# Attention and two expert networks on one core: first scores and last evictions moved across the branch, masks in two parts, three products moved between the last turns and values

## The chip, the cores and the metric

The kernel runs on one core of one Trainium2 chip. The time is device microseconds (us) of one execution; the smaller the better. TensorE is called PE here, its weight loads PEld, VectorE DVE, ScalarE ACT, GpSimd POOL and SyncE SP, as in the profile.

## What is computed

The input is q, k, v (2 batches, 8 heads, 768 positions, 64 per head) and the weights of two networks. The first stage is attention in which a row sees the first `n_sink` = 4 positions and the last `window` = 128; the second is a gated network of width 2048, the third a mixture of 4 experts of width 1024, all in float32.

```
keep = is_sink | ((rel >= 0) & (rel < window))
scores = np.where(keep, scale * q @ k.T, -1e9); a = exp(scores - max); a /= a.sum()
x = (a @ v) as 1536 tokens x 512
h = x @ w_in;  g = h * tanh(log1p(exp(h)));  x = g @ w_out
out = sum over 4 experts of p[:, e] * (relu(x @ w1[e]) @ w2[e])
```

## The kernel before

Every engine has a program of its own, written out by hand; semaphores tie them. All engines first run a short setup, then read a flag (`value_load`) that DVE computes from `n_sink` and `window`, and branch: the windowed attention (taken here) or a general one. Each path ends with its own copy of `networks`.

**Attention.** Two heads at a time (`ct` = 0 to 3) are worked in 24 units: unit u is one head's scores of 128 query rows in one batch. Four units make a group g (0 to 5 in a `ct`), so there are 24 groups. A unit passes PE (`score_of`, into one of four banks, `UP_BANK + u % 4`), DVE (`mask_scores`, adds the mask and finds the row minimum), ACT (`exponent`), and by groups DVE (`invert`), POOL (`normalise`), PE (`turn`, transposes), ACT (`copy_first`) and DVE (`copy_second`), PE (`values`), ACT and DVE (`take`: the result as a high part `x_hi` and a rest `x_lo`). PE's program for a period is scores of group g, `values` of group g - 3, `turn` of group g - 2. The first two query blocks of a batch need masks of 128 and 256 columns, the others 272 columns, in an even and an odd kind.

**First network.** PE makes 32 steps `up` (12 products of 128x512, 4 for each of three high/low combinations) and `down` (12 more) per 512 tokens and pass. Step s passes a chain of DVE and ACT between them: `start_gate` (DVE), `exponential` (ACT), `square` (DVE), `reciprocal` (ACT, two instructions), `finish_first` and `finish_second` (DVE, four instructions, the last counted by `g_done`), `gate_hi` (ACT), `gate_lo` (DVE, counted by `mish_lo`). `down` of step s waits for `mish_lo` s + 1. PE runs three `up` ahead (`LAG`); the first three are `start_up(0..2)`, made in the attention's code between the last groups, and `networks` begins with

```
                pe.wait_ge(x_lo_done, X_DONE)
                chunk(0, 0, False)
```

that is, a wait for the last `take` of the attention, then the fourth `up`. ACT's program after its last exponents is in this order: `copy_first` of group 4 of the last `ct`, three instructions that split weight tiles 3 and 4, `exponential(0)`, `take` of group 4, `copy_first` of group 5, `reciprocal(0)`, `take` of group 5; then `networks`, which splits tile 5 and then runs `gate_hi(0)`. DVE's is: `copy_second` 4, `start_gate(0)`, `square(0)`, `take` 4, `copy_second` 5, `finish_first(0)`, `finish_second(0)`, `start_gate(1)`, `take` 5, and in `networks` `gate_lo(0)`, `square(1)`, `start_gate(2)`.

**Experts.** PE alternates products (`L813`) and `tile_down` (`L887`); DVE's `evict` (L1673) adds a tile to the output's sum, six tiles in TILE_ORDER per step. Tile k may be written when the eviction of tile k - 4 is done. SP sends each of the last tiles out as soon as it is evicted, and waits for all of them.

## Time and profile before

| | us |
|---|---|
| median of 3 runs | 859.29 (858.17 to 859.41) |
| the profiled execution's own time | 859.52 |
| its span | 857.7 |
| PE busy | 844.3 (98%) |
| DVE busy | 606.3 (71%) |
| ACT busy | 401.9 (47%) |
| POOL busy | 169.3 (20%) |
| granted TensorE clock, mean | 0.999 |

The span begins with the first instruction and ends with the last; the time of a run is 1.82 us more than the span. The attention ends at about 97 us, the first network at about 360 us. Busy shares are averages over stages with different limits, so the stage in question has to be read by itself. In a timeline row the first number is the start, the second the duration, and in brackets stands how long the engine was idle before it and what the profile names as having ended that.

### The profile page before, as it was taken

The numbers are of one execution on the slowest core, as the hardware profiler recorded it, in microseconds if no ns is written. First come the engines' busy times: TensorE is split into PE (matmuls) and PEld (weight loads), VectorE is DVE, ScalarE is ACT, GpSimd is POOL, SyncE is SP. The second block draws the span as 40 slices with busy tenths as digits, with TensorE's granted clock in tenths as the row PEclk, the third lists the DMA queues.
The fourth block names the chain that finished last, engine by engine and source line by source line (L and its number), as shares of the span: only waits on it lengthen the run. The fifth ranks groups of instructions, "written<-read, shape, count | busy, mean of one in ns | idle before, by whom it ended". The sixth has DMA issues, their size and how long they took to land.

```text
span 857.7 us, 13864 instructions
## 1 busy us (share of the span) xinstructions
PE 844.3 (98%) x4512; PEld 730.1 (85%) x4512; DVE 606.3 (71%) x1173; ACT 401.9 (47%) x739; POOL 169.3 (20%) x255
## 2 busy tenths in 40 slices
PE   6999999999999999999999999999999999999997
PEld 4777888888888888899998999889989998899886
DVE  6888699888888989876566565565565655656655
ACT  5999764447754548754224324314314423432310
POOL 4777300001100112222022012112202202202100
PEclk9999999999999999999999999999999999999999
DMA  7355640003850005734055045135225315403303
GB/s 255 120 152 169 170 101 1 0 1 74 196 124 0 0 0 107 165 72 91 27 118 115 17 100 116 34 82 116 52 64 116 69 47 116 95 24 65 68 9 142
DMA packets 25191, 72.72 MB, mean 85 GB/s; under 512 B 4288, under 2 KB 5952, under 8 KB 25152
## 3 DMA queue, kind: packets, MB, share of 16 engines
q0 software_dynamic: 10720, 33.82, 21.8%
q1 hardware_dynamic: 14288, 38.04, 12.9%
q10 hardware_dynamic: 144, 0.39, 0.1%
q8 instruction: 17, 0.28, 0.1%
q14 instruction: 22, 0.18, 0.1%
HBM read 35.28 MB, written 3.15 MB: 45 GB/s over the span
## 4 chain that ended last, share of the span: by engine, by line
PE 97%; DVE 1%; ACT 1%; DMA 1%; issue 0%; DVEq 0%; ACTq 0%
PE banks L887 31%; PE banks L813 27%; PE banks L784 15%; PE banks L606 15%; PE banks L687 3%; PE banks L660 2%; PE banks L621 2%; PE banks L693 1%; DMA prm<-params 1%; ACT pool L982 0%; ACT prob_third L982 0%; DVE pool L1402 0%; PE banks L663 0%; DVE mask L1313 0%; DVE pool L1673 0%
## 5 line engine op out<-in xcount | busy, mean ns | idle before, releaser
L1673 DVE SCALAR_TENSOR_TENSOR pool<-banks,p_norm,pool 128x512 f32<-128x512 f32 x180 | 133.5, 748 | 66.7 <-PE banks L887 65.0
L887 PE MATMUL banks<-w_hi,g_lo 128*128 128x512 f32 x384 | 150.7, 392 | 0.0
L887 PE MATMUL banks<-w_lo,g_hi 128*128 128x512 f32 x384 | 150.5, 392 | 0.0
L887 PE MATMUL banks<-w_hi,g_hi 128*128 128x512 f32 x384 | 149.3, 389 | 0.0
L1203 ACT ACTIVATE g_hi<-pool 128x384 fp32r<-128x384 f32 x96 | 50.5, 526 | 190.8 <-DVE pool L1653 139.2
L813 PE MATMUL banks<-x_hi,w_lo 128*128 128x384 f32 x256 | 86.0, 336 | 0.0
L813 PE MATMUL banks<-x_hi,w_hi 128*128 128x384 f32 x256 | 85.9, 335 | 0.0
L813 PE MATMUL banks<-x_lo,w_hi 128*128 128x384 f32 x256 | 85.7, 335 | 0.0
L887 PEld LDWEIGHTS banks<-w_hi,g_lo 128*128 128x128 f32 x384 | 72.0, 188 | 15.1
L887 PEld LDWEIGHTS banks<-w_lo,g_hi 128*128 128x128 f32 x384 | 72.1, 188 | 13.9
L887 PEld LDWEIGHTS banks<-w_hi,g_hi 128*128 128x128 f32 x384 | 72.1, 188 | 13.6
L1197 ACT ACTIVATE g_hi<-banks 128x384 fp32r<-128x384 f32 x32 | 15.7, 491 | 131.4 <-PE banks L813 131.4
L519 POOL DMA_DIRECT2D w_lo<-w_sum x15 | 13.1, 875 | 323.3 <-ACT w_lo L1113 323.3
L784 PE MATMUL banks<-g_hi,w_hi 128*128 128x512 f32 x192 | 75.4, 393 | 0.2 <-DVE g_lo L1532 0.2
L606 PE MATMUL banks<-x_hi,w_hi 128*128 128x512 f32 (+1 forms) x192 | 75.0, 391 | 0.0
L784 PE MATMUL banks<-g_hi,w_lo 128*128 128x512 f32 x192 | 74.8, 390 | 0.0
L784 PE MATMUL banks<-g_lo,w_hi 128*128 128x512 f32 x192 | 74.8, 390 | 0.0
L606 PE MATMUL banks<-x_lo,w_hi 128*128 128x512 f32 (+1 forms) x192 | 74.8, 389 | 0.0
L606 PE MATMUL banks<-x_hi,w_lo 128*128 128x512 f32 (+1 forms) x192 | 74.7, 389 | 0.0
L1660 DVE SCALAR_TENSOR_TENSOR g_lo<-pool,g_hi 128x384 fp32r<-128x384 f32 x96 | 53.2, 555 | 21.6 <-ACT g_hi L1203 17.8
L959 ACT ACTIVATE pool<-pool,two 128x512 f32<-128x512 f32 x48 | 34.8, 724 | 69.9 <-DVE pool L1370 69.9
L1631 DVE TENSOR_TENSOR pool<-banks,pool 128x384 f32<-128x384 f32 x32 | 17.8, 557 | 53.6 <-ACT pool L1132 44.5
(142 smaller groups left out, 1770.0 us busy)
## 6 DMA issues: line engine op xcount, KB each, us to landing
w_raw<-weights SPq DMA_DIRECT2D x48, 512.0 KB, 4.3
w_lo<-w_raw POOLq DMA_DIRECT2D x48, 512.0 KB, 5.4
w_lo<-w_sum POOLq DMA_DIRECT2D x15, 384.0 KB, 4.0
pool<-kT SPq DMA_DIRECT2D x8, 400.0 KB, 5.1
pool<-v SPq DMA_DIRECT2D x8, 384.0 KB, 3.2
out<-pool SPq DMA_DIRECT2D x12, 256.0 KB, 2.2
pool<-qT SPq DMA_DIRECT2D x7, 384.0 KB, 4.2
w_lo<-pool POOLq DMA_DIRECT2D x2, 384.0 KB, 4.9
```

Source lines behind the costliest of these rows:

```text
L606: mm = pe.matmul(banks[:, 4 + f % H_RING, :], w[:, f, k * P:(k + 1) * P], x[:, k, ds(c * CHUNK, CHUNK)], start=(k == 0 and n == 0), stop=( ...
L621: mm = pe.matmul(bank[:, col:col + n], q_pair[rows, b, j * P:(j + 1) * P], k_pair[rows, b, key:key + n], start=True, stop=True)
L660: mm = pe.transpose(banks[:, TURN_BANK + n, P * (2 * h + k):P * (2 * h + k) + P], window_prob(u + h, WIDE)[:, col:col + P], ident[:, :])
L687: mm = pe.matmul(banks[D * h:D * h + D, out_bank, column], v_pair[:, b, kt, D * h:D * h + D], prob_T[:, slot, P * (2 * h + k):P * (2 * h + ...
L784: mm = pe.matmul(banks[:, i, :], w[:, f, lo:hi], g_slot(h, g), start=(f == 0 and n == 0), stop=(f == STEPS - 1 and n == 2), skip_group_che ...
L813: mm = pe.matmul(banks[:, bank, 0:HALF], w_cols(w, p2 * SLOT + at + k * P, P), x_part(lo, s, name)[:, k * HALF:(k + 1) * HALF], start=(fir ...
L887: mm = pe.matmul(banks[:, bank, :], g[:, s, f * SUP + at:f * SUP + at + P], w_cols(w, p2 * SLOT + DOWN_AT[f], DM), start=(f == 0 and n == ...
L959: act.activation(r_buf[:, s % 2, :], n_buf[:, s % 2, :], ACT.Ln, bias=two[:, 0:1]).then_inc(l_done, 1)
L1203: act.activation(relu_of(s, f, l), source, ACT.Relu).then_inc(relu_hi, 1)
L1631: dve.tensor_tensor(c12, bank(5 + s), p1_sum, ALU.add).then_inc(sum_done, 1)
L1660: dve.scalar_tensor_tensor(out=g_lo[:, s, at], in0=source, scalar=0.0, in1=g_hi[:, s, at].bitcast(f32), op0=ALU.max, op1=ALU.subtract).the ...
L1673: dve.scalar_tensor_tensor(out=to, in0=d_bank, scalar=share, in1=to, op0=ALU.mult, op1=ALU.add)\
```

## The change

Start. The first key and query loads of batch 0 are split: the first 256 columns of each on a semaphore `qk_first`, the rest on `qk_in[0]`. PE makes the scores of units 0 to 3 before it reads the flag, instead of after the branch. DVE makes only the masks of 128 and 256 columns and one narrow one before the branch; the even masks follow behind unit 3, the odd ones behind unit 5. The test of the two limits is made by other small instructions, as many as before. `rel`, from which masks are made, moves to `prob_third`, which is first overwritten in group 2. ACT copies the transposes of group 0 behind unit 9 instead of unit 11.

Attention to network. `start_up(0..2)` each move one place forward, and the last `values` now stands directly ahead of `networks`. `gate_hi(0)` moves ahead of the split of weight tile 5.

End. DVE's last six evictions move from the end of `networks` to behind the branch, shared by both paths.

```diff
-            for b, part in ((0, "k"), (0, "v"), (1, "q"), (1, "k"), (1, "v")):
+            sp.dma_start(k_pair[:, 0, 0:2 * P], kT[0, 0, :, 0:2 * P]).then_inc(qk_first, 16)
+            sp.dma_start(k_pair[:, 0, 2 * P:], kT[0, 0, :, 2 * P:]).then_inc(qk_in[0], 16)
+            for b, part in ((0, "v"), (1, "q"), (1, "k"), (1, "v")):
...
             def start_up(f):
-                pe.wait_ge(masked, CT * UNITS)
+                pe.wait_ge(masked, CT * UNITS - 3 + f)
...
+                start_up(0)
                 values(CT - 1, GROUPS_A - 3)
                 turn(CT - 1, GROUPS_A - 2)
-                start_up(0)
+                start_up(1)
                 values(CT - 1, GROUPS_A - 2)
                 turn(CT - 1, GROUPS_A - 1)
-                start_up(1)
+                start_up(2)
                 values(CT - 1, GROUPS_A - 1)
-                start_up(2)
...
+            pe.wait_ge(qk_first, 32)
+            for u in range(4):
+                score_of(u, 0, u // 2, banks[:, UP_BANK + u, :], attention_plan(True)[1], scored)
+            pe.wait_ge(ident_done, 2)
...
-                            if u % 4 == (3 if g % (QT // 2) else 1):
+                            if u % 4 == (1 if g % (QT // 2) == 0 or ct * GROUPS_A + g == 2 else 3):
...
-            act.dma_start(q_pair[:, 0, :], qT[0, 0, :, :]).then_inc(qk_in[0], 16)
+            act.dma_start(q_pair[:, 0, 0:2 * P], qT[0, 0, :, 0:2 * P]).then_inc(qk_first, 16)
+            act.dma_start(q_pair[:, 0, 2 * P:], qT[0, 0, :, 2 * P:]).then_inc(qk_in[0], 16)
...
-                        if s == 1:
+                        if s == 0:
                             gate_hi(0)
...
+            def even_masks():
+                mask_off(even, rel[:, 0:P], window_limit)
+                mask_off(even + P + SINKS, rel[:, P:], window_limit)
+            def odd_masks():
+                mask_off(odd, pos[:, :], sink_limit)
+                mask_off(odd + SINKS, rel[:, :], window_limit)
...
                     mask_scores(ct, 4 * g + 1)
+                    if early(ct, g, 2) and g == 1:
+                        odd_masks()
...
                     mask_scores(ct, 4 * g + 3)
+                    if early(ct, g, 1):
+                        even_masks()
...
                 pair_step(2 * PAIRS - 1, 1, E - 1, False)
-                for k in range(SUP_TILES):
-                    evict(2 * PAIRS - 1, 1, E - 1, False, k)
...
+            for k in range(SUP_TILES):
+                evict(2 * PAIRS - 1, 1, E - 1, False, k)
```

DVE at the start, from the first test of a limit to the first masked unit. L1402 before and L1417 of the changed kernel are `mask_scores`, `flag` is what all engines read. Before:

```order
L1313 TENSOR_SCALAR mask<-pos,lim 128x16
L1332 SCALAR_TENSOR_TENSOR ok<-lim,ok 128x1
L1336 CAST flag<-ok 128x1
L1313 TENSOR_SCALAR mask<-pool,lim 128x256
L1341 TENSOR_TENSOR mask<-mask 128x16 x2
L1313 TENSOR_SCALAR mask<-pool,lim 128x128 x2
L1313 TENSOR_SCALAR mask<-pool,lim 128x256
L1744 TENSOR_LOAD flag
L1745 COMPARE_AND_BRANCH
L1402 ISA pool,row_min<-banks,mask 128x128
```

and now:

```order
L1343 TENSOR_TENSOR ok<-ok 128x1
L1328 TENSOR_SCALAR mask<-prob_third,lim 128x256
L1347 CAST flag<-ok 128x1
L1351 TENSOR_TENSOR mask<-mask 128x16 x2
L1767 TENSOR_LOAD flag
L1768 COMPARE_AND_BRANCH
L1417 ISA pool,row_min<-banks,mask 128x128
```

The three masks that stood between the two narrow ones and the read of the flag are gone from there.

PE where the attention ends, behind the loop's last branch, with the semaphores that it waits for. L687 and L693 before (L694 and L700 now) are `values`, L660 and L663 (L667, L670) `turn`, L606 (L608) `up`, whose other eleven products are left out. Before:

```order
L707 COMPARE_AND_BRANCH
L687 MATMUL banks<-pool 64x128 [waits first_copied,x_lo_done,v_in1]
L687 MATMUL banks<-pool 64x128
L687 MATMUL banks<-pool 64x128 [waits second_copied]
L687 MATMUL banks<-pool 64x128 x3
L660 MATMUL banks<-ident,pool 128x128 [waits first_copied,prob_ready]
L660 MATMUL banks<-ident,pool 128x128 x3
L660 MATMUL banks<-ident,pool 128x128 [waits second_copied,prob_ready]
L660 MATMUL banks<-ident,pool 128x128 x2
L660 MATMUL banks<-ident,pool 128x128 [waits x_lo_done,sink_out,sinks_ready]
L663 MATMUL banks<-ident,pool 64x128
L606 MATMUL banks<-x_hi,w_hi 128x512 [waits w_lo_in0,x_lo_done,masked]
```

and now:

```order
L714 COMPARE_AND_BRANCH
L608 MATMUL banks<-x_hi,w_hi 128x512 [waits w_lo_in0,x_lo_done,masked]
...
L694 MATMUL banks<-pool 64x128 [waits first_copied,x_lo_done,v_in1]
L694 MATMUL banks<-pool 64x128
L694 MATMUL banks<-pool 64x128 [waits second_copied]
L694 MATMUL banks<-pool 64x128 x3
L667 MATMUL banks<-ident,pool 128x128 [waits first_copied,prob_ready]
L667 MATMUL banks<-ident,pool 128x128 x3
L667 MATMUL banks<-ident,pool 128x128 [waits second_copied,prob_ready]
```

The first `up` now stands ahead of the `values` of group 3 and of the `turn` of group 4, and so on by one place for the other two.

## Rows read from the trace of the kernel before

**Rows 1.** The page: shares of the chain that ended last, by engine.
```profile
PE 97%; DVE 1%; ACT 1%; DMA 1%; issue 0%; DVEq 0%; ACTq 0%
```

**Rows 2.** Busy time by stretch: from:to and length, PE, PEld, DVE, ACT, POOL.
```profile
16.00:85.00 69.00, 68.69 (x749) 52.96 (x748) 59.03 (x258) 62.86 (x208) 52.80 (x102) 1.00 0.51 147
...
98.00:200.00 102.00, 102.00 (x450) 83.74 (x449) 90.77 (x149) 55.29 (x85) 2.60 (x3) 1.00 0.14 37
```

**Rows 3.** Timeline of DVE at the start.
```profile
6.84 0.15 DVE L1336 CAST flag<-ok 128x1 int32<-128x1 f32 x1
6.91 0.34 DVE L1313 TENSOR_SCALAR mask<-pool,lim 128x256 f32<-128x256 f32 x1
...
7.47 0.74 DVE L1313 TENSOR_SCALAR mask<-pool,lim 128x128 f32<-128x128 f32 x3
...
9.10 0.29 DVE L1402 CUSTOM_DVE_ANT_0 pool<-banks,mask 128x128 f32<-128x128 f32 x1 [0.89 <-PE banks L621]
```

**Rows 4.** The chain that ended last, at the start: start, duration, what.
```profile
8.24 0.55 DVEq L1744
```

**Rows 5.** Timeline of the first groups.
```profile
10.94 0.44 DVE L1402 CUSTOM_DVE_ANT_0 pool<-banks,mask 128x272 f32<-128x272 f32 x1 [0.50 <-ACT pool L982]
...
11.67 0.17 DVE L1412 TENSOR_SCALAR row_den<-row_sum 128x4 f32<-128x4 f32 x1
...
14.35 2.43 POOL L451 TENSOR_TENSOR pool<-pool,row_den 128x272 f32<-128x272 f32 x4 [0.32 <-DVE row_den L1415]
...
15.48 0.29 PEld L621 LDWEIGHTS banks<-pool 64*128 64x128 f32 x2 [0.30 <-DVE row_min L1402]
...
16.46 0.66 PEld L687 LDWEIGHTS banks<-pool 128*64 128x64 f32 x12 [0.68 <-issue]
```

**Rows 6.** Timeline of PE where the attention ends.
```profile
85.74 0.88 PE L687 MATMUL banks<-pool 128*64 128x128 f32 x12 [0.71 <-ACT pool L993]
...
87.48 0.19 PEld L606 LDWEIGHTS banks<-x_hi,w_hi 128*128 128x128 f32 x1
...
90.45 0.42 PEld L687 LDWEIGHTS banks<-pool 128*64 128x64 f32 x8 [0.35 <-issue]
...
95.80 0.42 PEld L687 LDWEIGHTS banks<-pool 128*64 128x64 f32 x8 [0.35 <-issue]
...
97.26 0.19 PEld L606 LDWEIGHTS banks<-x_hi,w_hi 128*128 128x128 f32 x1 [0.17 <-issue]
```

**Rows 7.** Timeline of ACT and DVE in the same stretch.
```profile
87.24 0.60 ACT L993 ACTIVATE pool<-banks 128x512 f32<-128x512 f32 x1 [0.43 <-PE banks L660]
...
96.69 0.69 DVE L1396 SCALAR_TENSOR_TENSOR pool<-banks,pool 128x512 f32<-128x512 f32 x1
...
97.89 0.41 DVE L1422 TENSOR_TENSOR x_lo<-banks,x_hi 128x256 fp32r<-128x256 f32 x1
...
98.61 1.05 ACT L971 ACTIVATE w_lo<-w_raw 128x1024 fp32r<-128x1024 f32 x1
99.55 0.62 ACT L1086 ACTIVATE g_hi<-pool 128x512 fp32r<-128x512 f32 x1
...
100.07 0.62 ACT L955 ACTIVATE pool<-pool 128x512 f32<-128x512 f32 x1
```

**Rows 8.** Timeline of DVE and PE at the third step of the network.
```profile
113.01 0.69 DVE L1532 TENSOR_TENSOR g_lo<-pool,g_hi 128x512 fp32r<-128x512 f32 x1
...
113.76 0.50 PE L784 MATMUL banks<-g_hi,w_hi 128*128 128x512 f32 x1
```

**Rows 9.** Timeline of DVE and SP at the end.
```profile
846.92 0.75 DVE L1673 SCALAR_TENSOR_TENSOR pool<-banks,p_norm,pool 128x512 f32<-128x512 f32 x1
...
853.43 0.75 DVE L1673 SCALAR_TENSOR_TENSOR pool<-banks,p_norm,pool 128x512 f32<-128x512 f32 x1 [0.61 <-PE banks L887]
...
854.21 0.33 SPq L425 DMA_DIRECT2D out<-pool  x1
```

**Rows 10.** DMA issues of the line that writes the output, from the last two.
```profile
DMA to landing us min/median/max: 3.1/3.1/3.2
```

More of the change, by code:

```diff
@@ L292, in build @@
         probs_in = sem("probs_in")
+        qk_first = sem("qk_first")
+        full_scored = sem("full_scored")
         qk_in = [sem(f"qk_in{b}") for b in range(B)]
@@ L591, in _ @@
         def _(pe):
-            pe.wait_ge(ident_done, 2)
             def hidden_ready(s):
@@ L726, in score @@
                         pe.wait_ge(masked, ct * UNITS + u + 1 - FULL_SCORES)
-                    score_of(u, u // (2 * QT), u // 2 % QT, full_bank[u % FULL_SCORES], segments)
+                    score_of(u, u // (2 * QT), u // 2 % QT, full_bank[u % FULL_SCORES], segments,
+                             full_scored if early(ct, u, 4) else scored)
                 def turn(ct, u):
@@ L1431, in mask_scores @@
                     w = width[j]
+                    if early(ct, u, 7) and u in (0, 4, 6):
+                        dve.wait_ge(mask_ready, {0: 5, 4: 7, 6: 9}[u])
                     dve.wait_ge(scored, ct * UNITS + u + 1)
@@ L1465, in period @@
                     mask_scores(ct, 4 * g + 3)
+                    if early(ct, g, 1):
+                        even_masks()
                     if first_half:
@@ L1490, in mask_scores @@
                     to = scores_f[:, u % FULL_SCORES, :]
-                    dve.wait_ge(scored, ct * UNITS + u + 1)
+                    if early(ct, u, 4):
+                        dve.wait_ge(full_scored, u + 1)
+                    else:
+                        dve.wait_ge(scored, ct * UNITS + u + 1)
                     if not early(ct, u, FULL_SCORES):
@@ L1526, in full_attention, with evict @@
                 start_gate(1)
+            def evict(it, s, e, first, k):
+                dve.wait_ge(tile_done, SUP_TILES * it + k + 1)
+                tile = TILE_ORDER[k]
+                to, d_bank = out_acc(s, tile), banks[:, (2 * s + k) % 4, :]
+                token = s * SUP_TILES + tile
+                share = p_norm[:, ds(e, 1), token:token + 1].rearrange("p a n -> p (a n)")
+                if first:
+                    dve.tensor_scalar(to, d_bank, share, None, ALU.mult).then_inc(evicted, 1)
+                else:
+                    dve.scalar_tensor_tensor(out=to, in0=d_bank, scalar=share, in1=to, op0=ALU.mult, op1=ALU.add)\
+                       .then_inc(evicted, 1)
             def networks():
@@ L1661, in relu_rest @@
                                              op0=ALU.max, op1=ALU.subtract).then_inc(relu_lo, 1)
-                def evict(it, s, e, first, k):
-                    dve.wait_ge(tile_done, SUP_TILES * it + k + 1)
-                    tile = TILE_ORDER[k]
-                    to, d_bank = out_acc(s, tile), banks[:, (2 * s + k) % 4, :]
-                    token = s * SUP_TILES + tile
-                    share = p_norm[:, ds(e, 1), token:token + 1].rearrange("p a n -> p (a n)")
-                    if first:
-                        dve.tensor_scalar(to, d_bank, share, None, ALU.mult).then_inc(evicted, 1)
-                    else:
-                        dve.scalar_tensor_tensor(out=to, in0=d_bank, scalar=share, in1=to, op0=ALU.mult, op1=ALU.add)\
-                           .then_inc(evicted, 1)
                 def pair_step(it, s, e_before, first_before):
```

37 lines of the change are left out of this document (16 added, 21 removed).

## The prediction

> **What bounds the kernel now.** I read the chain that ended last first. 97% of it is PE [rows 1], so an edit is worth what it gives or takes on PE, and the other engines matter where PE waits for them. The second view is busy time by stretch: between 98 and 200 us PE is busy all of the time and DVE for 90.77 of 102 us [rows 2], so a DVE that starts late there catches up slowly. The third is the timeline at the three places that the change touches. At the start the path is DVE's: its masks run to 8.21 us [rows 3], then it reads the flag (0.55 us [rows 4]), and its first masked unit starts at 9.10 [rows 3]. From 16.46 us, where PE turns to its first `values` [rows 5], PE works through, period after period. Where the attention ends PE has one real gap, 0.71 us ahead of the `values` of group 3, which wait for ACT's copy [rows 6]. And at the third step of the network the gate chain is just in time: the `gate_lo` that the third `down` needs starts at 113.01 and ends at 113.70, and PE's `down` starts at 113.76 [rows 8]. That chain has no slack. This is the reading on which most depends.
>
> **The start.** Before the flag DVE's small instructions stay nearly as many, and the 256-column mask (0.34 us [rows 3]) moves ahead of the flag; in exchange one narrow mask and one step of the dependent tests leave. I take the flag to stay where it is, at 6.85 us [rows 3]. What leaves is the block of three masks, 0.74 us together, that begins at 7.47 [rows 3], and the wait for it. DVE now reaches the flag's read behind two narrow instructions (0.26 us together before), at 7.2. From the start of that read to the first masked unit it is 9.10 - 8.24 = 0.86 us [rows 3, 4]. So the first unit is masked at 8.05, 1.05 us earlier. PE's four scores must be there by then. They need a third of the q and k loads that they waited for before, and I take them as hidden.
>
> The masks are not gone, they come later. Behind unit 3 stand two of 128 columns. The block of three shows 0.20 us for one that is followed by another, (0.74 - 0.34) / 2 [rows 3]; the second counts with its whole length, about 0.28, because unit 4 waits for it, and then the next instruction has to be released: 0.05 us between neighbours that wait for nothing, 0.31 from the end of the flag's read to the first unit [rows 3, 4], and I take 0.25. That makes 0.73. Before, DVE was idle at this place for 0.50 [rows 5], so 0.23 are lost. Behind unit 5 stand 16 and 256 columns, some 0.33 us. `invert` of group 0, at 11.67 before [rows 5], comes at 11.67 - 1.05 + 0.23 + 0.33 = 11.18, and what is left of the gain is 0.5 to 0.55 us. ACT's exponents from unit 6 on follow DVE by that.
>
> ACT's copy of group 0 goes ahead of two exponents and no longer holds PE. PE loads the last weights of group 3's scores at 15.48 for 0.29 us, and then stands for 0.68 us until it starts `values` at 16.46 [rows 5]. Now it can go on: 15.48 - 0.52 + 0.29 + 0.05 = 15.3. The start gains 16.46 - 15.3, almost 1.2 us; I take **1.1**. It holds only if POOL follows. POOL normalises group 1 from 14.35 for 2.43 us [rows 5], now from 13.83 to 16.26. PE's `turn` of that group comes behind 0.81 us of `values` and wants POOL's second half only for its own second half, at about 16.6. The cover is 0.35 us. Bounds: 0.5, if DVE and ACT hold PE all along, and 1.5.
>
> The Trainium skill, "TensorE: Matmul & The Clock Gate", Part 1, has it that a PE that was idle runs at half rate until activity releases its clock. By it, earlier scores would bring the full clock sooner and the gain could be nearer its upper bound. The profile's granted clock, 0.999 as a mean, does not show a slow start.
>
> **Attention to network.** The gap of 0.71 us goes, since an `up` fills it [rows 6]. An `up` takes 90.45 - 87.48 = 2.97 us there, with the issue time around it [rows 6]. So each `turn` and `values` behind it is later by 2.95 - 0.71 = 2.2 us against the rest of the kernel. Who waits for the late ones?
> - PE itself. The last `values` began at 95.80 and an `up` followed at 97.26 [rows 6], which covered the `take`: its DVE half ended at 97.89 + 0.41 = 98.30 [rows 7]. Now `networks` waits for that directly, 1.04 us and the way of the semaphore, 1.2. Against the gap filled PE is 0.5 us late at its fourth `up`.
> - ACT has its copy of group 4 (87.24 before [rows 7]) ahead of three weight splits and `exponential(0)`. The copy now waits for a `turn` that is 2.2 us later; ACT stands idle, and the exponential comes later too, although its `up` is ready earlier. The early product brings nothing.
> - DVE has `finish_first(0)` behind `copy_second` of group 5, which waits for the late `turn`. The last instruction of the gate, 96.69 [rows 7], comes at 98.9 and ends at 99.6.
> - `gate_hi(0)` stood at 99.55 behind the split of tile 5, with `exponential(1)` right behind it at 100.07 [rows 7]. Now it stands ahead of the split, at about 99.85, once the last `take` and the gate are done; then 0.52 for itself (100.07 - 99.55) and 0.94 for each of the two splits (99.55 - 98.61 [rows 7]), and `exponential(1)` is at 102.25, 2.2 us late.
> - From there to the third `gate_lo` the chain is ACT and DVE alone, in the order that it had. So that ends at 113.70 + 2.2 = 115.9, and the third `down`, 113.76 before [rows 8], starts at 115.95. On PE these are 1.2 us at the wait for the `take` and 1.7 at the second and third `down`, less the 0.71 of the filled gap. The first two are one loss: had PE not stood at the `take`, it would stand longer at the `down`.
>
> Behind that, DVE, 89% busy in this stretch [rows 2], gains on PE and PE waits no more. The place costs **2.2 us**. Bounds: 0.5, if the gate chain has slack after all, and 2.4.
>
> **The end.** The last six evictions started from 846.92 to 853.43 [rows 9]; now DVE takes its jump ahead of them. Before, it made the jump behind 853.43 + 0.75 = 854.18 and within the span, which ends at 857.7, so the jump is no longer than 3.5 us, and the first eviction starts at 850.4 at the latest. The tiles come 0.61 + 0.75 = 1.36 us apart [rows 9], so the bank that it frees is wanted two tiles and one product ahead of the last eviction, at 850.7. PE is not held. Six evictions of 0.75 us, back to back, would end at 854.9, 0.7 us late: the bound of a loss. The gain is bounded too: the last output transfer is issued at 854.21 and lands 3.1 us later [rows 9, 10], so at most 0.35 us of the tail can be DVE's. I take 0, because a jump like the one at the start (0.31 us with what follows it) costs nothing.
>
> The Trainium skill, "Runtime: NRT & Kernel Launch", "Instruction fetch mechanics", says that a taken branch to a far target must first fetch the page there. By it the jump would be nearer to its bound than to 0.31 us; the sum would still be 0 up to a jump of 2.8.
>
> **Sum.** -1.1 + 2.2 + 0 = +1.1 us. The profiled execution took 859.52, so it would be 860.6; the median of the runs shown was 859.29, 0.23 less, and from that I forecast 860.4. What a measurement of this kernel can tell from no change is about 0.2%, 1.7 us.
>
> **The rivals.**
> - The gate chain has slack, and only the wait for the `take` counts: -1.1 + 0.5, 858.7 us. For it: the first gate starts from an earlier `up`. Against it: 0.06 us between `gate_lo` and `down` [rows 8].
> - Slower: the start gives nothing, because the later masks and ACT, 62.86 of 69 us busy over the attention [rows 2], hold PE to its old pace, and the transition's 2.2 us stand alone: 861.5 us, slower by 0.26%. For it: half of the gain is given back at `invert`, and POOL's cover is 0.35 us. Against it: PE's 0.68 us ahead of the first `values` [rows 5] were ACT's copy, which is out of the way. It decides from a gain of less than 0.5 us.
> - Faster: the gap goes, the start gains and nothing new waits: -1.1 - 0.7, 857.5 us. It needs a `take` that is over when PE asks for it, against the 1.04 us that it took [rows 6, 7].
>
> **How the numbers follow.** The forecast (both terms within 0.4 us) has a chance of 0.5, slack in the gate chain 0.15, no gain at the start 0.22, nothing waits 0.07, anything else 0.06. The range spans the first three and the runs' own spread (858.17 to 859.41 before): 858.3 to 861.7. Slower by over 0.2% is over 861.0: most of the third case and a little of the first, 0.23. Faster is under 857.6: half of the fourth and a little of the rest, 0.06. Within is what remains, 0.71.
>
> **What would show it.** First masked unit at 8.05 us, `invert` at 11.2, first `values` at 15.3. Where the attention ends, no gap ahead of the `values` of group 3; ACT idle for 2.5 to 3 us ahead of its copy of group 4; PE idle for 1.2 us ahead of the fourth `up`, then about 0.6 and 1.1 us ahead of the second and third `down`, against a `gate_lo`. The time from the last product to the end as before. I am wrong if PE's first `values` starts at 16 or later, or if no `down` waits.

## The result

The changed kernel took **862.07 us** (median of 8 runs, 859.95 to 863.46), the kernel before 859.11 (858.15 to 859.41) beside it on the same chip: a ratio of 1.0035, 95% interval 1.0022 to 1.0047. A second comparison gave 861.19 (859.15 to 863.29, 11 runs) and 1.0021 (1.0011 to 1.0032). I had forecast 860.4 and a range of 858.3 to 861.7: the first median lies 0.4 us outside it, the second inside. The kernel became slower by 2 to 3 us, and its runs scatter over 4 us, those of before over about 2.

### The profile after

The execution profiled took 861.65 us (span 859.8). First the page, the chain that ended last by engine, which answers to [rows 1], and two groups of its section 5 (busy time and mean, then idle time before them and who ended it):

```profile
PE 97%; ACT 1%; DVE 1%; DMA 0%; issue 0%; SPq 0%
...
L798 PE MATMUL banks<-g_hi,w_hi 128*128 128x512 f32 x192 | 75.4, 393 | 1.3 <-DVE g_lo L1570 1.3
L608 PE MATMUL banks<-x_hi,w_hi 128*128 128x512 f32 (+1 forms) x192 | 75.1, 391 | 1.2 <-DVE x_lo L1437 1.0
```

PE is the bound as before; new are 1.3 us of wait ahead of `down` (L798) and 1.2 ahead of `up` (L608), most of it for a `take`. Now the three places. The timeline of DVE at the start, which answers to [rows 3, 5]:

```profile
4.09 0.17 DVE L1320 CAST prm_f<-prm 128x2 f32<-128x2 uint32 x1 [2.28 <-DMA prm<-params]
...
6.48 0.29 DVE L1417 CUSTOM_DVE_ANT_0 pool<-banks,mask 128x128 f32<-128x128 f32 x1 [0.67 <-DVE mask L1351]
...
8.36 0.44 DVE L1417 CUSTOM_DVE_ANT_0 pool<-banks,mask 128x272 f32<-128x272 f32 x1 [0.22 <-PE banks L623]
...
9.49 0.17 DVE L1427 TENSOR_SCALAR row_den<-row_sum 128x4 f32<-128x4 f32 x1
```

The first masked unit is at 6.48 us, 2.62 earlier than before, where I had 1.05. More than half of that is one row: the parameters are there at 4.09, in the kernel before at 5.51:

```profile
5.51 0.17 DVE L1305 CAST prm_f<-prm 128x2 f32<-128x2 uint32 x1 [3.70 <-DMA prm<-params]
```

But PE does not turn this into time. Its timeline at the start, in this execution:

```profile
6.92 5.18 PE L623 MATMUL banks<-pool 64*128 64x272 f32 x16 [0.30 <-DVE row_min L1417]
12.03 1.54 PE L667 MATMUL banks<-ident,pool 128*128 128x128 f32 x6
13.50 1.65 PE L623 MATMUL banks<-pool 64*128 64x128 f32 x8
15.08 1.55 PE L694 MATMUL banks<-pool 128*64 128x128 f32 x12
16.56 1.23 PE L667 MATMUL banks<-ident,pool 128*128 128x128 f32 x8
...
17.83 1.19 PE L623 MATMUL banks<-pool 64*128 64x272 f32 x8
```

and of the same kernel in the execution profiled in the second comparison (861.37 us):

```profile
11.43 1.08 PE L667 MATMUL banks<-ident,pool 128*128 128x128 f32 x6
12.44 1.53 PE L623 MATMUL banks<-pool 64*128 64x128 f32 x8
13.90 0.88 PE L694 MATMUL banks<-pool 128*64 128x128 f32 x12
14.70 1.09 PE L667 MATMUL banks<-ident,pool 128*128 128x128 f32 x8
...
15.83 1.19 PE L623 MATMUL banks<-pool 64*128 64x272 f32 x8
```

The same 12 matmuls of `values` take 1.55 us in the one and 0.88 in the other. In the first PE works at half pace until about 16.5 us. In the second it is at full pace at 11.43 us at the latest: its six transposes there take 1.08 us, in the first at 12.03 they take 1.54. The last row of each, the scores of group 4, is the place to compare; in the kernel before it is this:

```profile
18.43 1.19 PE L621 MATMUL banks<-pool 64*128 64x272 f32 x8
```

So the start gains 0.60 us in the one and 2.60 in the other. The granted clock reads 1.00 in both stretches, the level of 2.4 GHz: that column does not show the half pace, only the durations do.

The transition, which answers to [rows 6 to 8]: ACT, then DVE, then PE.

```profile
89.07 0.60 ACT L1007 ACTIVATE pool<-banks 128x512 f32<-128x512 f32 x1 [2.86 <-PE banks L667]
...
92.41 0.61 ACT L969 ACTIVATE pool<-pool 128x512 f32<-128x512 f32 x1
...
99.49 0.62 ACT L1101 ACTIVATE g_hi<-pool 128x512 fp32r<-128x512 f32 x1
...
101.91 0.62 ACT L969 ACTIVATE pool<-pool 128x512 f32<-128x512 f32 x1
```

```profile
99.73 0.41 DVE L1437 TENSOR_TENSOR x_lo<-banks,x_hi 128x256 fp32r<-128x256 f32 x1
...
114.76 0.69 DVE L1570 TENSOR_TENSOR g_lo<-pool,g_hi 128x512 fp32r<-128x512 f32 x1
```

```profile
100.20 0.50 PE L608 MATMUL banks<-x_hi,w_hi 128*128 128x512 f32 x1 [1.04 <-DVE x_lo L1437]
...
109.02 0.50 PE L798 MATMUL banks<-g_hi,w_hi 128*128 128x512 f32 x1 [0.37 <-DVE g_lo L1570]
...
115.51 0.50 PE L798 MATMUL banks<-g_hi,w_hi 128*128 128x512 f32 x1 [0.73 <-DVE g_lo L1570]
```

The fourth `up` and the second `down` start in the kernel before at these times, without a wait:

```profile
100.15 0.39 PE L606 MATMUL banks<-x_hi,w_hi 128*128 128x512 f32 x1
...
108.31 0.39 PE L784 MATMUL banks<-g_hi,w_hi 128*128 128x512 f32 x1
```

The third `down` starts at 115.51 against 113.76 [rows 8], 1.75 later; with the 0.60 gained at the start the transition has cost 2.35 us. It is lost in three steps: 0.65 up to the fourth `up`, 0.66 more up to the second `down`, 1.04 more up to the third. And PE is busy for 99.87 of the 102 us from 98 on, before for all of them [rows 2].

The end. DVE, SP's landings for the twelve output transfers (with the durations of their issues), and the last product on PE:

```profile
851.00 3.50 DVE L1563 SCALAR_TENSOR_TENSOR pool<-banks,p_norm,pool 128x512 f32<-128x512 f32 x5 [2.32 <-PE banks L901]
855.11 0.75 DVE L1563 SCALAR_TENSOR_TENSOR pool<-banks,p_norm,pool 128x512 f32<-128x512 f32 x1 [0.61 <-PE banks L901]
```

```profile
L429 SPq DMA_DIRECT2D out<-pool x12: 332/332/352, 836.6 to 855.9; - x12
...
DMA to landing us min/median/max: 2.0/2.6/3.6
```

```profile
854.68 0.39 PE L901 MATMUL banks<-w_hi,g_lo 128*128 128x512 f32 x1
```

Five evictions run back to back behind the jump, which held the first for 2.32 us. None of them is late for PE. But their transfers now come in a bunch: from 852.5 to 856.0 the DMA engines are busy for 0.96 of the time, in the same place of before, counted from the last product, for 0.60 (windows; the two columns at the end are DMA share and GB/s):

```profile
852.50:856.00 3.50, 2.57 (x12) 1.79 (x10) 2.73 (x4) 0.00 (x0) 0.00 (x0) 1.00 0.96 356
```

```profile
850.83:854.33 3.50, 2.56 (x12) 1.79 (x10) 2.14 (x3) 0.00 (x0) 0.00 (x0) 1.00 0.60 220
```

From the start of the last product to the end of the span it is 859.8 - 854.68 = 5.12 us, before 857.7 - 853.01 = 4.69. In the second comparison's execution it is 6.85, and SP's own rows show why:

```profile
852.01 2.01 SPq L429 DMA_DIRECT2D out<-pool  x1
...
L429 SPq DMA_DIRECT2D out<-pool x12: 332/333/2011, 834.6 to 854.5; - x12
...
DMA to landing us min/median/max: 2.0/2.4/4.6
...
852.75 0.39 PE L901 MATMUL banks<-w_hi,g_lo 128*128 128x512 f32 x1
```

One issue of an output transfer stands for 2.01 us where the others take 0.33; the last one, whose eviction ended at 853.93, is issued at 854.5. That is about 0.6 us late; the rest of the longer tail is its landing, up to 4.6 us after the issue, before at most 3.2.

### The profile page after: what moved, and what is told of

Same layout as the page of the kernel before. It is cut to its first block, busy times and chain, and to the rows that moved or that the text cites. A ratio compares the mean times of both kernels' runs of the same rounds, so it can differ in the third digit from the quotient of the medians.

```text
span 859.8 us, 13868 instructions
## 1 busy us (share of the span) xinstructions
PE 847.2 (99%) x4512; PEld 731.0 (85%) x4512; DVE 606.1 (70%) x1173; ACT 401.8 (47%) x739; POOL 169.5 (20%) x255
## 4 chain that ended last, share of the span: by engine, by line
PE 97%; ACT 1%; DVE 1%; DMA 0%; issue 0%; SPq 0%
PE banks L901 31%; PE banks L827 27%; PE banks L798 15%; PE banks L608 14%; PE banks L623 3%; PE banks L667 3%; PE banks L694 3%; PE banks L700 1%; DMA pool<-kT 0%; ACT pool L973 0%; ACT pool L975 0%; ACT w_hi L982 0%; ACT w_lo L985 0%; PE banks L670 0%; ACT g_hi L1101 0%
## 5 line engine op out<-in xcount | busy, mean ns | idle before, releaser
L798 PE MATMUL banks<-g_hi,w_hi 128*128 128x512 f32 x192 | 75.4, 393 | 1.3 <-DVE g_lo L1570 1.3
L608 PE MATMUL banks<-x_hi,w_hi 128*128 128x512 f32 (+1 forms) x192 | 75.1, 391 | 1.2 <-DVE x_lo L1437 1.0
L798 PE MATMUL banks<-g_lo,w_hi 128*128 128x512 f32 x192 | 74.8, 390 | 0.0
L798 PE MATMUL banks<-g_hi,w_lo 128*128 128x512 f32 x192 | 74.8, 390 | 0.0
L608 PE MATMUL banks<-x_hi,w_lo 128*128 128x512 f32 (+1 forms) x192 | 74.7, 389 | 0.0
L608 PE MATMUL banks<-x_lo,w_hi 128*128 128x512 f32 (+1 forms) x192 | 74.7, 389 | 0.0
```

The lines of the kernel that those rows point to most:

```text
L608: mm = pe.matmul(banks[:, 4 + f % H_RING, :], w[:, f, k * P:(k + 1) * P], x[:, k, ds(c * CHUNK, CHUNK)], start=(k == 0 and n == 0), stop=( ...
L798: mm = pe.matmul(banks[:, i, :], w[:, f, lo:hi], g_slot(h, g), start=(f == 0 and n == 0), stop=(f == STEPS - 1 and n == 2), skip_group_che ...
```

## The experiments

All kernels compute the whole reference. Each time stands beside that of the kernel before on the same chip; "tail" is the time from the start of the last product to the end of the span in the profiled execution.

### Each part alone, and the change again

**start_only**: the changed kernel with the other two parts undone. 

> The start of the change alone: split loads, four scores ahead of the branch, masks in two parts, the early copy; the order at the attention's end and the last evictions are as before. Theory 1 (the changed kernel's trace): PE gains 0.6 us at its 17.8 us scores in the profiled execution, and more or less in others, because PE's products run at half pace for a variable time: median between -1.5 and +1.5 us against before, with runs 2 us or more apart, where before they are 1.3 us apart. Theory 2 (the prediction): -1.1 us, and runs as close together as before.

**middle_only**: the kernel before with the three `start_up` calls one place earlier and `gate_hi(0)` ahead of the split. 

> Only the three early products one place forward and gate_hi(0) ahead of the split of tile 5. Theory 1 (gate chain without slack, as predicted): +2.2 to +2.4 us, runs as close together as before; the fourth up waits 1.0 to 1.2 us and the second and third down wait together 1.2 to 1.7 us. Theory 2 (the chain has slack): +0.5 us.

**end_only**: the kernel before with this behind the branch:

```diff
-                for k in range(SUP_TILES):
-                    evict(2 * PAIRS - 1, 1, E - 1, False, k)
+            for k in range(SUP_TILES):
+                evict(2 * PAIRS - 1, 1, E - 1, False, k)
```

> Only the last six evictions behind the branch. Theory 1: DVE is held at the jump for 2 to 3.5 us, the output transfers of the last tiles pile up, and the last one lands later: +0.3 to +0.5 us, more in runs in which the jump takes longer. Theory 2 (the prediction): 0 within 0.3 us.

**after_again**: the changed kernel once more. 

> The changed kernel once more, for a second profiled execution beside the other three on the same chip. Theory 1 (variable half pace of PE at the start): the time of the profiled execution and the moment at which six transposes take 0.9 instead of 1.5 us move together, about half a us for each us. Theory 2 (the jump at the end varies): executions differ between the last product and the end instead. Median +2.5 to +3.2 us against before.

Measured against 858.89 us for the kernel before: the start 857.01 (0.9978, 0.9969 to 0.9987), so -1.9; the transition 861.56 (1.0029, 1.0017 to 1.0040), so +2.7; the end 859.91 (1.0007, 0.9998 to 1.0016), so +1.0, in two clusters of runs, near 859.1 and near 860.0. So the start is larger than my term for it, and the transition is near its term. The end's interval touches no change; that the end is not nothing rests on the runs below. The sum, +1.8, is under the whole's +2.3 and +3.0, and no run shows where the rest comes from.

### no_end: the change without the moved evictions

> The changed kernel with the last six evictions put back inside the branch; the start and the attention-to-network part stay as changed. Parts run alone so far gave 857.0 (start), 861.6 (attention to networks), 859.9 (evictions behind the branch), against 858.9 for the kernel before. Theory A, the evictions behind the branch cost what I had put at nothing: this kernel comes at 858.9 - 1.9 + 2.7 = 859.7, some 1 to 2 us under the changed kernel, its runs lie within about 1 us of each other, and the last eviction ends about 3.6 us before the span's end. Theory B, the start and the transition work against each other, and the evictions are innocent: it comes at 861 or above and scatters over 3 us as the changed kernel did.

860.55 us (858.96 to 861.12), 1.0015 (1.0006 to 1.0024), against 859.12. No theory has it whole. The median lies between the two, and nothing is left above 861.2, where the changed kernel had 11 of its 19 runs. The tail of its profiled execution is 4.61 us, as before the change. And yet the runs spread over 2.2 us (the kernel before over 1.7 beside it): in that execution PE kept the half pace late (scores of group 4 at 17.56), in after_again, with the same start, it did not (15.83). So the end is one source of the scatter, the start another.

### take_late and gate_early: which wait makes the transition's loss

Both are built on no_end. take_late moves one wait on PE:

```diff
-                pe.wait_ge(x_lo_done, X_DONE)
+                pe.wait_ge(masked, CT * UNITS)
                 chunk(0, 0, False)
...
+                        if f == LAG and not before:
+                            pe.wait_ge(x_lo_done, X_DONE)
```

> The same as no_end, with TensorE's wait for the last take moved from ahead of the fourth up-projection to ahead of the first down-projection (the fourth up-projection then waits only for the last masked score). Theory A, the chain of gate 0 and 1 on ScalarE and VectorE sets the pace of the first three down-projections: the 1.2 us wait for the take vanishes and reappears at the second down-projection as about 1.8 us instead of 0.6; the third is as late as before and the time is that of no_end within 0.3 us. Theory B, the wait for the take is a cost of its own: the kernel is 1.0 to 1.2 us faster than no_end.

gate_early leaves PE alone and reorders ACT (below) and DVE in the same sense:

```diff
-                copy_first(CT - 1, GROUPS_A - 2)
                 split_tile_neg(EARLY - 2)
                 split_tile_hi(0, EARLY - 1, None)
-                split_tile_neg(EARLY - 1)
                 exponential(0)
-                take_after(CT - 1, GROUPS_A - 2)
-                copy_first(CT - 1, GROUPS_A - 1)
+                copy_first(CT - 1, GROUPS_A - 2)
                 reciprocal(0)
+                split_tile_neg(EARLY - 1)
+                take_after(CT - 1, GROUPS_A - 2)
+                copy_first(CT - 1, GROUPS_A - 1)
+                gate_hi(0)
+                exponential(1)
                 take_after(CT - 1, GROUPS_A - 1)
```

> The same as no_end, with ScalarE and VectorE in another order at the transition: splits and exponential(0) ahead of the copy of group 10's turn, reciprocal(0) right behind that copy, gate_hi(0) and exponential(1) ahead of the last take; on VectorE start_gate(0) and square(0) ahead of the second copy of group 10, gate_lo(0) and square(1) ahead of the last take. Theory A, the transition loses only because the gates' chain stays behind TensorE's earlier up-projections: gate_hi(0) starts about 3 us and exponential(1) about 3.9 us earlier, the waits at the second and third down-projection (0.4 and 0.7 to 1.1 us) vanish, about 1.0 us of wait for the take stays, and the kernel comes 1.5 to 2.0 us under no_end, near 857.9. Theory B, the early up-projections cost for another reason (operands, banks): the same as no_end.

take_late: 859.89 us (1.0013, 1.0004 to 1.0022), gate_early: 857.99 (0.9990, 0.9981 to 0.9999). The median of take_late is 0.66 under no_end's, more than theory A's 0.3 and less than theory B's 1.0; that of gate_early is 2.6 under it. Such medians mix executions that reach full pace early and late, so the profiled ones are the better measure: in both, as in after_again, PE was at full pace by 11.5 us. PE's waits from 84 to 125 us (in all, times, longest), take_late and then gate_early:

```profile
PE banks L798 <- DVE g_lo L1572: 2.2, 2, 1.4
```

```profile
PE banks L608 <- DVE x_lo L1445: 0.9, 1, 0.9
```

With the wait for the `take` moved, its 1.0 us reappears at the second `down`, which now waits for 1.4; the last product starts at 852.72 against 852.75 in after_again. With the gates moved, both waits at `down` are gone, ACT runs the first exponential 3.9 us before its place under the old order, and the last product starts at 851.00, 1.75 earlier:

```profile
86.51 0.63 ACT L976 ACTIVATE pool<-pool 128x512 f32<-128x512 f32 x1 [0.30 <-DVE pool L1381]
...
94.65 0.63 ACT L971 ACTIVATE g_hi<-pool 128x512 fp32r<-128x512 f32 x1 [1.51 <-DVE pool L1419]
...
96.04 0.63 ACT L976 ACTIVATE pool<-pool 128x512 f32<-128x512 f32 x1 [0.76 <-DVE pool L1381]
```

By the places in the profiled executions that is theory A in both: the gate chain sets the loss, and the wait for the `take` is part of it, not added to it. The early up-projections are then still worth nothing against start_only (last product at 850.38).

### bunch_only and hold_three: output transfers in a bunch, evictions untouched

bunch_only, on the kernel before (hold_three has 3 in place of 4):

```diff
                 for n, tile in enumerate(TILE_ORDER):
+                    if s == 1 and n == 0:
+                        sp.wait_ge(evicted, SUP_TILES * (2 * PAIRS - 3 + s) + 4)
                     sp.wait_ge(evicted, SUP_TILES * (2 * PAIRS - 3 + s) + n + 1)
```

> The kernel before, with one wait more on SyncE's queue: the last six output transfers are held until four of the last six evictions are done, so that four are issued back to back, as after the jump of the changed kernel, while VectorE's evictions run as before with no jump ahead of them. Theory A, what the moved evictions cost is the bunching of the outputs at the end (in one execution of the changed kernel one issue took 2.01 us where the others took 0.33 us, and the last transfer landed 1.7 us late): this kernel is 0.3 to 1.5 us slower than the kernel before, with some runs over 1 us slower, and an issue above 1 us shows in slow ones. Theory B, the bunch is absorbed (the last two transfers go as before, queue idle by then): the same within 0.3 us, and the cost of the moved part lies in the jump itself or in the code behind it.

> The kernel before with SyncE's last six output transfers held until three (in bunch_only: four) of the last six evictions are done, so that three are issued back to back at about 850 us, the moment at which the moved evictions' bunch begins; VectorE is untouched and nothing lies behind the branch. Theory A, the moved evictions cost by the backlog of 256 KB transfers and an issue that is stuck in it: this kernel costs about what the moved evictions cost alone (+0.4 to +1.0 us), with an issue above 1 us in the slow runs. Theory B, only the four held until 851.2 us in bunch_only were too late for the last transfer, and the moved evictions cost through the jump: no cost (within 0.3 us of the kernel before).

bunch_only: 860.40 us (859.85 to 860.93) against 859.12, 1.0015 (1.0006 to 1.0024), +1.3. hold_three: 859.66 against 858.85, 1.0008 (0.9999 to 1.0017), +0.8; its interval touches no change, as that of end_only does, and the two agree. DVE's last eviction is where it was in both. The issues and landings of hold_three, beside a longest issue of 0.50 us in the kernel before:

```profile
L426 SPq DMA_DIRECT2D out<-pool x12: 332/333/1075, 834.6 to 853.9; - x12
...
DMA to landing us min/median/max: 2.0/2.5/3.6
```

So the transfers' bunch alone, with no jump ahead of it, costs about what the moved evictions cost alone, and in bunch_only the interval excludes no change. Theory A, except that bunch_only has no issue above 1 us (longest 0.77, tail 5.95): the backlog costs without it.

### end_act: the last transfer from another queue

On end_only, ScalarE issues the very last transfer, behind its own branch, and SP leaves it out:

```diff
+            act.wait_ge(evicted, SUP_TILES * (2 * PAIRS - 1))
+            act.dma_start(out.rearrange("(t p) n -> t p n", p=P)[SUP_TILES + TILE_ORDER[-1], :, :],
+                          out_acc(1, TILE_ORDER[-1])).then_inc(out_done, 16)
```

> The kernel before with the last six evictions behind the branch (859.9 us alone, 859.0 to 860.7, against 858.9), and the very last output transfer issued by ScalarE's queue instead of SyncE's. Theory A, the last transfer is late because its issue stands behind the bunch of five on SyncE's queue: the kernel is back at 859.1 or below, with no run above 859.8. Theory B, the transfers share the engines whoever issues them, so that the last one lands when the backlog of 256 KB pieces is through: the same as the part alone, 859.6 to 860.2.

859.36 us, 9 of 11 runs from 859.27 to 859.68, the slowest 860.84, against 858.89 (1.0007, 0.9998 to 1.0016). It lies between the two and settles nothing. In its profiled execution one of SP's issues stood for 1.62 us and the last transfer, issued by ACT at 854.6, landed 3.1 us later as ever: the tail was 4.73.

### whole_loads: where the start's gain comes from

The start part with the first q and k in one transfer each; the loads in two parts of the change are undone, q's on ACT in the same way as k's on SP, and the first scores wait for both:

```diff
-            sp.dma_start(k_pair[:, 0, 0:2 * P], kT[0, 0, :, 0:2 * P]).then_inc(qk_first, 16)
-            sp.dma_start(k_pair[:, 0, 2 * P:], kT[0, 0, :, 2 * P:]).then_inc(qk_in[0], 16)
+            sp.dma_start(k_pair[:, 0, :], kT[0, 0, :, :]).then_inc(qk_in[0], 16)
```

> The start part alone, but with the first q and k loaded whole, as in the kernel before; the first scores wait for both. Theory A, most of the gain comes from the scores' standing ahead of the branch and from the masks in two parts, and the parameters' 4.04 us is chance: parameters land at 4.0 to 4.2, the first scores start at about 6 us when the whole loads are in, the kernel is 0.5 to 1.2 us slower than the start part. Theory B, the parameters land early because the transfer behind them in the queue is smaller: they land at 5.2 to 5.5 again, the first masked score starts 1.2 to 1.4 us later, and the kernel is 1.0 to 1.6 us slower than the start part, at about -0.5 against the kernel before.

858.88 us against 858.85, 1.0001 (0.9992 to 1.0010): the whole gain is gone. Parameters and first scores:

```profile
5.19 0.17 DVE L1318 CAST prm_f<-prm 128x2 f32<-128x2 uint32 x1 [3.39 <-DMA prm<-params]
```

```profile
6.60 6.97 PE L622 MATMUL banks<-pool 64*128 64x128 f32 x24 [6.60 <-DMA pool<-kT]
```

Theory B. The parameters are at 4.02 to 4.14 us in all thirteen profiled executions with the loads in two parts and at 5.19 to 5.93 in all seven with whole loads, though their own transfer is issued first in all, at 0.75 us. The first scores, too, start 1.6 us later. Which of the two counts for more this run does not tell.

It leaves something open. The first masked unit is at 7.58 us here, 1.5 earlier than in the kernel before, and the first scores 1.2 earlier, and still the median gains nothing. The execution profiled is the slowest of its eleven (860.20), and in it the half pace goes on past 18 us, where eight transposes take 1.09 at full pace:

```profile
18.03 1.53 PE L666 MATMUL banks<-ident,pool 128*128 128x128 f32 x8
```

So it does not show what an execution with whole loads and an early full pace would gain.

### The half pace at the start

after_warm (on the changed kernel), start_warm (on start_only) and gate_warm (on gate_early) put eight transposes on PE ahead of the first scores, long_warm and long_again (on start_only) and after_long (on the changed kernel) eleven; start_again is start_only once more:

```diff
+            pe.wait_ge(ident_done, 2)
+            for n in range(8):
+                pe.transpose(banks[:, TURN_BANK, 0:P], ident[:, :], ident[:, :])
             pe.wait_ge(qk_first, 32)
```

> The whole changed kernel, with eight transposes of the identity into a bank that nobody reads yet, put on TensorE ahead of the first scores (the identity is there at 2.3 us, the first scores start at 4.97). So far the scores of group 4 started at 15.83 us in four profiled executions of kernels with the new start and at 17.6 to 17.8 us in two, where TensorE's rows kept twice the duration until about 16.8 us. Theory A, in those two TensorE worked at half pace because it had been idle until 4.97 us, and how long that lasts differs between executions: with work ahead of it the rows reach full pace before 10 us in every execution, the scores of group 4 start at 15.8 or a little earlier, and the kernel comes 0.8 to 1.5 us under the changed kernel, near 860.0 to 860.5, with what spread the last transfers give. Theory B, the half pace has nothing to do with what TensorE did before: no change in time or spread (861.2 to 862.1).

> The start part alone (857.0 us, 856.4 to 858.2) with the same eight transposes ahead of the first scores. Theory A: the slow executions near 858 vanish, the median comes to 856.2 to 856.8, and the first 16 wide scores take less than 4.6 us. Theory B: the same as the start part alone within 0.3 us.

> gate_early (start, early up-projections, reordered gates; 858.0 us, 857.0 to 859.5) with the same eight transposes. Theory A: the spread shrinks to about 1 us and the median comes to 856.8 to 857.3. Theory B: 858.0 and the same spread. In both the transition is still worth nothing against the start part alone, since its wait for the take (0.9 us) is larger than the gap that it fills (0.7 us).

> The start part alone with eleven transposes of the identity ahead of the first scores instead of eight, so that TensorE has no gap of 0.6 us between them and the scores (which then start at about 5.1 us). Theory A, eight did not end the half pace since the gap undid them: the first wide scores run at full pace, group 4 starts at 15.8 or earlier in every execution, the median is at or under that of start_again, spread 1 us. Theory B, the end of the half pace does not follow from what TensorE does in the first 5 us: the same spread of 2 to 3 us, the median within 0.5 us of start_again.

> The start part alone once more, unchanged (857.01 us, 856.4 to 858.2, in its first comparison; with eight transposes ahead 857.95, 856.7 to 859.4). Theory A, the fast and the slow start are chance of each execution and not of a kernel: runs lie between 856.4 and 859.4 as those of the two together, with a median of 857.0 to 858.0. Theory B, the transposes themselves cost 0.9 us: the median is 857.0 again with nothing above 858.3.

> The whole changed kernel with eleven transposes of the identity ahead of the first scores. Theory A, the changed kernel's spread of 859.2 to 863.5 us is the product of two things, TensorE's half pace at the start (given back up to 2 us) and the last transfers (0 to 2 us), and eleven transposes take the first away: the median is about 858.9 - 1.9 + 2.2 + 1.0 = 860.2, no run is above 861.5, and the scores of group 4 start at about 15.9 us. Theory B, the even start in the comparison with eleven transposes was chance: the median stays at 861.0 to 862.1, with runs above 862.

> The start part with eleven transposes once more, as the version that is to beat both kernels. Theory A, the transposes even the start out: 857.0 within 0.3 us again, nothing above 858.3. Theory B, chance: the median and the slowest run lie with those of the start part alone (857.0 and 857.4; 858.2 and 858.7).

The scores of group 4 and the tail are those of the profiled execution.

| kernel | us (runs) | kernel before | scores of group 4, us | tail, us |
|---|---|---|---|---|
| after_warm | 860.95 (860.21 to 862.53) | 858.89 | 16.85 | 6.74 |
| start_warm | 857.95 (856.70 to 859.39) | 858.89 | 17.54 | 4.20 |
| gate_warm | 857.64 (857.12 to 858.64) | 858.89 | 15.82 | 4.78 |
| long_warm | 857.00 (856.65 to 857.99) | 858.85 | 15.87 | 4.85 |
| start_again | 857.36 (856.55 to 858.70) | 858.85 | 15.89 | 4.37 |
| after_long | 861.01 (859.43 to 862.63) | 859.00 | 15.88 | 6.67 |
| long_again | 857.06 (856.37 to 858.48) | 859.00 | 17.08 | 4.36 |

Eight transposes do not help: two of the three executions profiled reached full pace late, and the transposes themselves took 0.25 us each, half pace. Eleven, with no gap behind them, looked like the cure in long_warm, but in long_again's profiled execution the half pace lasted until about 15 us all the same:

```profile
2.39 2.61 PE L786 MATMUL banks<-ident 128*128 128x128 f32 x11 [2.39 <-POOL ident L445]
4.93 1.65 PE L623 MATMUL banks<-pool 64*128 64x128 f32 x8
6.88 5.17 PE L623 MATMUL banks<-pool 64*128 64x272 f32 x16 [0.30 <-DVE row_min L1420]
11.98 1.54 PE L667 MATMUL banks<-ident,pool 128*128 128x128 f32 x6
```

and after_long scatters as the changed kernel does. Theory B in these, then, and start_again, the same code as start_only, shows a spread like that of start_warm: when PE reaches full pace differs between executions of one kernel. My theory that PE's idle time ahead of the scores sets it has fallen, as far as work of up to 2.6 us can tell. What does set the moment stays open.

It may not be chance alone. In the six profiled executions with the old start the scores of group 4 come 10.59 to 10.63 us after the first scores. In the fourteen with scores ahead of the branch (whole_loads among them) it is 10.8 to 10.95 us in eight and 11.9 to 13.0 in six. Six executions are too few to say that the old start never has the long half pace, but in them it did not occur.

## Why the prediction was wrong, and where it was right

- **The transition, +2.2: right, by its steps.** The places that I gave, less the 0.60 us by which this execution was early: ACT idle for 2.86 us ahead of its copy (2.5 to 3 forecast), `gate_hi(0)` at 99.49 + 0.60 = 100.09 (99.85), `exponential(1)` at 102.51 (102.25), third `down` at 116.11 (115.95); lateness gained up to the fourth `up` 0.65 (0.5), the second `down` 0.66 (0.6), the third 1.04 (1.1). The waits that the rows name there are shorter (1.04, 0.37 and 0.73). Of the gap of 0.71 us, which I had as gone, 0.21 stays, ahead of the first early `up` at 84.64. The transition cost 2.35; alone the last product was 2.04 later (855.05 against 853.01) with a start that was 0.23 early, so 2.27, and the median 2.7. That the wait for the `take` and those at the `down` "are one loss" is what take_late shows, and that the lateness goes through ACT's and DVE's order is what gate_early shows.
- **The end, 0: wrong, and what takes the time past the forecast.** The step that failed is "The gain is bounded too: the last output transfer is issued at 854.21 and lands 3.1 us later", and with it "the sum would still be 0 up to a jump of 2.8". I asked when the last eviction would end, and that was right: DVE was held for 2.32 us, PE waited for nothing, the sixth eviction started 0.43 us after the last product, before 0.42. I took the last transfer's 3.1 us as its own property. It is that of a transfer with little queued ahead of it. With five transfers of 256 KB issued close together from 851.78 on, and then the sixth, the tail grew from 4.69 to 5.12 and 6.85 us; in the four profiled executions of the whole change (two of them with transposes ahead) it was 5.12, 6.85, 6.74 and 6.67, in the twelve with neither moved evictions nor held transfers 4.18 to 4.85. (end_only's own was 4.63, in a run of its lower cluster, end_act's 4.73.) The term was 0 and measured +1.0 alone (0.8 for the bunch alone), and in the whole change 0.4 to 2.2 in the profiled ones. Without the moved evictions, in no_end, the change came at 860.55, +1.4, where +1.1 was forecast for the other two parts; that it came so near is in part luck, since alone the start gained more than its term and the transition lost more. The Trainium skill, "Runtime: NRT & Kernel Launch", "Instruction fetch mechanics", has a taken branch to a far target fetch the page there first. The 2.32 us that DVE was held are in line with it; at the start it was 0.31, and no run shows that either was a fetch.
- **The start, -1.1: mis-sized twice, in opposite senses.** The step "I take the flag to stay where it is, at 6.85 us" failed: the flag was written at 5.43, since the parameters landed 1.42 us earlier. The mask part was right as far as the first masked unit (1.2 of its 2.62, forecast 1.05), and the four scores were ready, as I had taken them to be. But I had costed the loads in two parts at nothing, and whole_loads, which lacks just them, gained nothing. So that the mask part alone gives PE any time is not shown. Second, "The profile's granted clock, 0.999 as a mean, does not show a slow start" was true of the column and no evidence: PE starts at half pace all the same, and the transposes show full pace at 11.43 us in one execution of the changed kernel and only behind 16.5 in the other. The Trainium skill, "TensorE: Matmul & The Clock Gate", Part 1, has a PE that starts at half rate and a moment that differs from run to run. The rows of this case agree with both, but not with the size of the difference: the page gives plus or minus 0.5 us, here it is about 5 us in one and the same kernel. What it does to the sum is in rows: 2.60 gained or 0.60, alone a median of 1.9 and 1.5. The first `values` was forecast at 15.3; it came at 15.08 by the slow pace and at 13.90 by the fast, each time for reasons that were not mine.
- **The sum.** -1.1 + 2.2 + 0 = +1.1 was forecast. Counted by the start of the last product and the tail the profiled execution has -0.60 + 2.27 + 0.43 = +2.1 (spans: 859.8 - 857.7), and after_again's has -2.60 + 2.34 + 2.16 = +1.9 (859.6 - 857.7). The range missed by 0.4 us because it held no loss at the end at all (its own bound, 0.7, did not enter it), and no scatter beyond that of the kernel before.
- **The rivals.** The slower one came near in its time, 861.5, but not by its mechanism: the start gained, and POOL was not later (it started group 1 at 12.17, before at 14.35 [rows 5]). Slack in the gate chain is refuted by take_late and by middle_only's +2.7, where it would have been +0.5.

**The version that beats both** is the start part alone: 857.01 and 857.36 us, ratios 0.9978 (0.9969 to 0.9987) and 0.9988 (0.9979 to 0.9997); with eleven transposes 857.00 and 857.06, 0.9979 both times (0.9970 to 0.9988).

## What to carry to other kernels

Work put earlier on the bounding engine was worth nothing here while the engines that use its result kept their order: move the whole chain, or expect the gap that you fill to come back as a wait a few steps on. At the end of a kernel ask when the last transfer is *issued* and what is still in the queue ahead of it, not only when the last result is ready. And at the start compare the same matmuls' durations, not the clock column, and look at several executions before a gain of 1 us is put down to an edit.

## What the runs showed of the hardware that I had not expected

- A transfer of 2 KB, issued first, was in use at 4.02 to 4.14 us or at 5.19 to 5.93, depending on whether the q and k loads behind it came in two parts or whole.
- Of the issues of output transfers in a bunch, single ones stood for 1.08, 1.62, 1.98, 2.01 and 2.06 us instead of 0.33; with none bunched the longest was 0.65.
- TensorE worked at half pace until past 16.5 us in one execution and past 18 in another (whole_loads), where others were at full pace at 11.4 to 11.5, with a granted clock of 1.00 in the rows of the stretch. Work of 2.0 or 2.6 us ahead of the first scores did not reliably end it sooner.
